# Two linear-attention heads at a time, then an MLP and a mixture of experts: weight halves and first rows made by VectorE, zero rows spread over pairs, 16-bit rank marks

## What is computed

```python
# attention: 4 x 8 heads, 576 positions, head size 64, 128 features
phi(x) = concat(exp(p), exp(-p)),  p = x @ w_phi - max|x @ w_phi|
kv = phi(k)^T v;  z = sum over positions of phi(k)
x  = (phi(q) kv) / (phi(q) z + 1e-6)              # 2304 tokens x 512
# MLP: 512 -> 2048 -> 512
h = x @ w_in;  y = (h * clip(h + 3, 0, 6) / 6) @ w_out
# mixture: 8 experts 512 -> 1024 -> 512, each token to its best expert
e = argmax(y @ w_gate); out = softmax(...)[e] * sigmoid(y @ w_output_gate)[e] * relu(y @ w1[e]) @ w2[e]
```

## Time and profile before

| | |
|---|---|
| median of three runs | 861.08 us |
| the profiled execution, its own time | 853.36 us |
| its span, first to last instruction | 851.8 us |
| TensorE matmul busy | 812.8 us, 95% |
| VectorE busy | 566.5 us, 67% |
| ScalarE busy | 388.9 us, 46% |
| GpSimd busy | 204.0 us, 24% |
| mean granted TensorE clock | 0.99 |

### The profile page before, as it was taken

One profiled execution on the slowest core, in us unless ns is written; L12 is line 12 of the kernel. 1 busy time (PEld: TensorE's weight loads), 2 busy tenths in 40 slices (PEclk: granted clock), 3 DMA queues, 4 the chain that ended last, 5 costly groups with the idle time before them and its releaser, 6 DMA issues.

```text
span 851.8 us, 19379 instructions
## 1 busy us (share of the span) xinstructions
PE 812.8 (95%) x7122; PEld 511.2 (60%) x7123; DVE 566.5 (67%) x1142; ACT 388.9 (46%) x843; POOL 204.0 (24%) x217
## 2 busy tenths in 40 slices
PE   6999989997899999999999999999998999999995
PEld 5666656664455455455455455456677777777773
DVE  5777878885887988998898898854732453222221
ACT  5877678883556546555555555533211121111110
POOL 4446579991000001001001001010121222111100
PEclk9999999999899999999999999999999999999998
DMA  7456866646263864955765855485263852565610
GB/s 230 148 195 195 250 198 205 196 139 213 89 233 133 262 213 173 260 223 174 246 222 197 234 222 210 136 343 178 100 220 105 321 208 79 227 223 221 223 65 13
DMA packets 67453, 164.41 MB, mean 193 GB/s; under 512 B 28614, under 2 KB 32966, under 8 KB 60736
## 3 DMA queue, kind: packets, MB, share of 16 engines
q1 hardware_dynamic: 61472, 146.74, 50.9%
q0 software_dynamic: 5760, 16.80, 5.6%
q10 hardware_dynamic: 160, 0.07, 0.0%
HBM read 114.16 MB, written 47.55 MB: 190 GB/s over the span
## 4 chain that ended last, share of the span: by engine, by line
PE 63%; DVE 18%; issue 7%; DMA 6%; ACT 2%; SPq 2%; POOL 1%; DVEq 0%; ACTq 0%; POOLq 0%
PE ps L900 14%; PE ps L995 13%; PE ps L983 13%; PE ps L889 12%; DVE arena L1556 3%; PE ps L749 3%; DVE u_mx L1529 3%; DMA recs<-rec 2%; PE ps L805 2%; PE ps L777 2%; DVE arena L1299 2%; DVE relu L1612 2%; DMA arena<-split 1%; PE ps L973 1%; DVE y_words L1521 1%
## 5 line engine op out<-in xcount | busy, mean ns | idle before, releaser
L889 PE MATMUL ps<-arena,w_in_sb 128*128 128x384 f16 x1152 | 201.8, 327 | 1.9 <-issue 1.9
L900 PE MATMUL ps<-w_out_sb,arena 128*128 128x512 f16 x576 | 172.7, 382 | 10.6 <-DVE stage L1617 10.6
L889 PEld LDWEIGHTS ps<-arena,w_in_sb 128*128 128x128 f16 x1152 | 112.5, 98 | 84.1 <-issue 3.6
L983 PE MATMUL ps<-x_t,arena 128*128 128x128 f16 x2112 | 121.5, 219 | 2.7 <-issue 2.7
L1276 ACT ACTIVATE x_t<-ps 128x512 f16<-128x512 f32 x54 | 31.6, 596 | 201.1 <-PE ps L983 175.8
L983 PEld LDWEIGHTS ps<-x_t,arena 128*128 128x128 f16 x2112 | 119.3, 98 | 6.6 <-issue 3.3
L995 PE MATMUL ps<-arena,x_t 128*128 128x512 f16 x528 | 117.9, 379 | 0.0
L900 PE MATMUL ps<-w_out_sb,stage 128*128 128x512 f16 x288 | 110.0, 382 | 0.0
L1248 ACT ACTIVATE arena<-relu 128x384 f16<-128x384 f32 x96 | 50.0, 520 | 116.3 <-DVE relu L1612 115.1
L900 PEld LDWEIGHTS ps<-w_out_sb,arena 128*128 128x128 f16 x576 | 55.8, 98 | 72.0 <-issue 15.0
L1099 ACT ACTIVATE arena<-ps,arena 128x128 f32<-128x128 f32 x288 | 79.8, 396 | 34.0 <-DVE arena L1301 24.1
(11 more groups left out here) (209 smaller groups left out, 949.7 us busy)
## 6 DMA issues: line engine op xcount, KB each, us to landing
arena<-split SPq DMA_DIRECT2D x36, 1024.0 KB, 5.8
arena<-in_moe_w SPq DMA_DIRECT2D x16, 2048.0 KB, 13.2
split<-arena SPq DMA_DIRECT2D x16, 2048.0 KB, 7.4
arena<-in_qkt SPq DMA_DIRECT2D x15, 576.0 KB, 6.6
stage<-in_moe_w_in SPq DMA_DIRECT2D x16, 512.0 KB, 5.4
stage<-in_moe_w_out SPq DMA_DIRECT2D x16, 512.0 KB, 6.4
x_t<-rows POOLq DMA_DIRECT2D x27, 257.0 KB, 3.0
y_words<-recs SPq DMA_DIRECT2D x32, 144.0 KB, 3.0
```

The source lines that it names most:

```text
L889: last = nc.tensor.matmul(ps[:, HB[f % GB], 0:BN], w_in_sb[:, lw, c, f * P:(f + 1) * P], xt[:, a, lx, c, :], start=c == 0 and lw + lx == 0 ...
L900: last = nc.tensor.matmul(ps[:, YB + r, :], g_sb[lg_][:, f % GB, r * P:(r + 1) * P], w_out_sb[:, lw, f, :], start=f == 0 and lg_ + lw == 0 ...
L983: last = nc.tensor.matmul(ps[:, bank, f % 4 * P:(f % 4 + 1) * P], w1_sb[b][:, lw, c, f * P:(f + 1) * P], xgt[:, a, lx, c, :], start=c == 0 ...
```

## The change

1. The high half of `w_in` is made by VectorE right before the low half (`piece_lo_of`, w = 0), no longer by GpSimd. In pair 14 this pair of operations moves from behind the scales to behind group 1 of the differences.
2. The first rows' high half is made by VectorE in one operation (`first_x`), no longer by ScalarE in two; the low half is one operation too. The last piece of `w_out` comes behind them.
3. `copy_low(u)` waits for the denominators of pair u-2 instead of u-1 (one semaphore for each buffer). VectorE takes the reciprocals of pair u-2 ahead of `copy_high(u)`, not behind it. ScalarE's loop starts two pairs later, the pairs before it are written out.
4. The zero rows go out one DMA in each pair from 8 to 15.
5. At the transition SyncE loads the second expert unit behind `rec_out(13)`, `rec_in(13)` and `den_over(15)`, not ahead of them.
6. GpSimd normalises up to pair 11 (before: 10). VectorE takes the reciprocals of pair 14 in chunk 1 of block 0 and those of pair 15 in chunk 4, with normalisations 12 and 13; 14 and 15 are in chunk 14.
7. The rank matmuls take a triangle, a square of ones and `onehot` in 16 bits.

```diff
-                if u == PAIRS // 2 - 1:
+                e = u - (PAIRS - E)
+                if e == 0:
                     sp.wait_ge(consts_made, 2)
-                    for e in range(E):
-                        sp.dma_start(rows[e * REGION:e * REGION + P, :], zrow).then_inc(pads_stored, 16)
+                if e >= 0:
+                    sp.dma_start(rows[e * REGION:e * REGION + P, :], zrow).then_inc(pads_stored, 16)
...
-            for m in range(2):
-                load_unit(0, m, m)
+            load_unit(0, 0, 0)
             rec_out(PAIRS - 3)
             rec_in(PAIRS - 3)
             den_over(PAIRS - 1)
+            load_unit(0, 1, 1)
...
             def last_pair():
                 sums_second(PAIRS - 1)
-                piece_hi_of(PAIRS - 1, 1)
-                normalise(PAIRS - 1 - BEHIND, 0)
+                for u in range(PAIRS - 1 - BEHIND, PAIRS - LAST):
+                    normalise(u, u % 2)
...
-                nc.tensor.matmul(ps[:, LB, 128:128 + BT * E], tri[:], rhs, start=True, stop=True)
-                nc.tensor.matmul(ps[:, LB, 192:192 + BT * E], ones[:], rhs, start=True, stop=True).then_inc(ranks_done, 1)
+                nc.tensor.matmul(ps[:, LB, 128:128 + BT * E], tri16[:], rhs, start=True, stop=True)
+                nc.tensor.matmul(ps[:, LB, 192:192 + BT * E], ones16[:], rhs, start=True, stop=True).then_inc(ranks_done, 1)
...
-                if not isinstance(u, int) or u > 0:
-                    act.wait_ge(den_moved, u * 16)
+                if not isinstance(u, int) or u > 1:
+                    act.wait_ge(den_moved[a], (u - a) * 8)
...
             def pair_out(u, a):
-                copy_high(u, a)
                 if not isinstance(u, int) or u > 1:
                     reciprocals(u - 2, a)
+                copy_high(u, a)
...
+                dst, cols = (w_in_flat, w_out_flat)[w], bass.ds((u - PAIRS // 2) * Q, Q)
+                if w == 0:
+                    dve.wait_ge(stage_loaded[a], (u - a) * 16 + 32)
+                    nc.vector.tensor_scalar(dst[:, 0, cols], stage[:, a, 0, :], s_up[:, 0:1], None, ALU.mult).then_inc(piece_hi, 1)
...
                 differences(u + 1, 1 - a, 1)
+                piece_lo_of(u, a, 0)
                 max_over_rows(1, 1)
                 differences(u + 1, 1 - a, 2)
                 max_of(1, slice(3, 4))
                 pair_out(u, a)
                 x_scales()
-                for w in range(2):
-                    piece_lo_of(u, a, w)
-                first_x_lo()
+                first_x()
+                piece_lo_of(u, a, 1)
...
+            def first_x():
+                dve.wait_ge(x_ready, DC)
+                nc.vector.tensor_scalar(xt[:, 0, 0], x_t[:, :, 0:BN], s_up[:, 3:4], None, ALU.mult).then_inc(xs_hi, 1)
+                x_lo(0, 0)
...
                     if f == 1 and not post:
-                        normalise(PAIRS - 5, 1)
-                        normalise(PAIRS - 4, 0)
+                        reciprocals(PAIRS - 2, 0)
+                    if f == 4 and not post:
+                        reciprocals(PAIRS - 1, 1)
+                        for u in range(PAIRS - LAST, PAIRS - 2):
+                            normalise(u, u % 2)
+                    if f == 14 and not post:
                         for u in range(PAIRS - 2, PAIRS):
-                            reciprocals(u, u % 2)
-                    if f == 4 and not post:
-                        normalise(PAIRS - 3, 1)
-                        normalise(PAIRS - 2, 0)
-                    if f == 14 and not post:
-                        normalise(PAIRS - 1, 1)
+                            normalise(u, u % 2)
```

More of the change, by code:

```diff
@@ L39 @@
 QUARTER = S // 4
-REP, WIDE, BEHIND = 32, 4, 5
+REP, WIDE, BEHIND, LAST = 32, 4, 5, 4
 GROUPS = [(8, 1), (0, 4), (4, 4)]
@@ L97, in moe_program @@
         ones = sb("ones", [P, P])
-        tri = sb("tri", [P, P])
+        ones16 = sb("ones16", [P, P], F16)
+        tri16 = sb("tri16", [P, P], F16)
         x_t = sb("x_t", [P, DC, N])
@@ L199, in moe_program @@
         r_b = sb("r_b", [P, BT, E])
-        onehot = sb("onehot", [P, BT, E])
+        onehot = sb("onehot", [P, BT, E], F16)
         r_s = sb("r_s", [P, 4, BT])
@@ L251, in moe_program @@
         high_copied = sem("high_copied")
-        den_moved = sem("den_moved")
+        den_moved = [sem(f"den_moved{a}") for a in range(2)]
         rec_made = sem("rec_made")
@@ L357, in pair_loop @@
             first()
-            both(0, 0, 0)
-            both(1, 1, 0)
-            with eng.Fori(1, PAIRS // 4) as i:
+            for u in range(4):
+                both(u, u % 2, 0)
+            with eng.Fori(2, PAIRS // 4) as i:
                 both(i * 2, 0, 0)
@@ L578, in later_constants @@
                 step(nc.gpsimd.tensor_copy(ident16[:], ident[:]))
-                step(nc.gpsimd.affine_select(out=tri[:], in_=ones[:], compare_op=ALU.is_ge, fill=0.0, base=-1,
+                step(nc.gpsimd.tensor_copy(ones16[:], ones[:]))
+                step(nc.gpsimd.affine_select(out=tri16[:], in_=ones16[:], compare_op=ALU.is_ge, fill=0.0, base=-1,
                                         pattern=[[1, P]], channel_multiplier=-1))
@@ L614, in normalise, with both @@
                 nc.gpsimd.tensor_tensor(x_of(u, 0, S), x_of(u, 0, S), rec_wide[:, bass.ds(u % WIDE * S, S)], ALU.mult).then_inc(x_ready, 1)
-            def both(u, a, phase):
+            def both(u, a):
                 sums_second(u)
-                if phase:
-                    piece_hi_of(u, a)
                 if u >= BEHIND:
@@ L633, in _ @@
             sums_first(1)
-            for u in range(1, PAIRS // 2):
-                both(u, u % 2, 0)
-            for u in range(PAIRS // 2, PAIRS - 1):
-                both(u, u % 2, 1)
+            for u in range(1, PAIRS - 1):
+                both(u, u % 2)
             last_pair()
@@ L1130, in x_hi @@
             def x_hi(n, b):
-                if isinstance(n, int) and n == 0:
-                    act.wait_ge(scale_step, X_UP)
-                    act.wait_ge(projected, PAIRS * 6)
-                    act.wait_ge(x_ready, DC)
-                else:
-                    first = isinstance(n, int) and n == 1
-                    act.wait_ge(x_ready, 2 * DC if first else PAIRS - BEHIND)
-                    if not first:
-                        act.wait_ge(x_last, BEHIND)
-                if isinstance(n, int) and n == 0:
-                    nc.scalar.activation(xt[:, b, 0, 0:2], x_t[:, 0:2, 0:BN], ACT.Copy, scale=s_up[:, 3:4]).then_inc(xs_half, 1)
-                    nc.scalar.activation(xt[:, b, 0, 2:DC], x_t[:, 2:DC, 0:BN], ACT.Copy, scale=s_up[:, 3:4]).then_inc(xs_hi, 1)
-                else:
-                    nc.scalar.activation(xt[:, b, 0], x_t[:, :, bass.ds(n * BN, BN)], ACT.Copy, scale=s_up[:, 3:4]).then_inc(xs_hi, 1)
+                first = isinstance(n, int) and n == 1
+                act.wait_ge(x_ready, 2 * DC if first else PAIRS - LAST)
+                if not first:
+                    act.wait_ge(x_last, LAST)
+                nc.scalar.activation(xt[:, b, 0], x_t[:, :, bass.ds(n * BN, BN)], ACT.Copy, scale=s_up[:, 3:4]).then_inc(xs_hi, 1)
             def parts(b):
@@ L1453, in x_scales @@
                 nc.vector.tensor_scalar(s_y[:], s_y[:], 1.0 / CG, None, ALU.mult).then_inc(x_scale, 1)
-            def first_x_lo():
-                for k, hi in ((0, xs_half), (2, xs_hi)):
-                    dve.wait_ge(hi, 1)
-                    last = nc.vector.scalar_tensor_tensor(out=xt[:, 0, 1, k:k + 2], in0=x_t[:, k:k + 2, 0:BN], scalar=s_up[:, 3:4],
-                                                          in1=xt[:, 0, 0, k:k + 2], op0=ALU.mult, op1=ALU.subtract)
-                last.then_inc(xs_lo, 1)
+            def first_x():
+                dve.wait_ge(x_ready, DC)
+                nc.vector.tensor_scalar(xt[:, 0, 0], x_t[:, :, 0:BN], s_up[:, 3:4], None, ALU.mult).then_inc(xs_hi, 1)
+                x_lo(0, 0)
             def x_lo(n, b):
```

16 lines of the change are left out of this document (3 added, 13 removed).

## The result

The changed kernel takes 852.27 us (median of 8 runs, 848.0 to 855.06) and the kernel before, run beside it, 859.88 us (8 runs, 857.72 to 862.28): a ratio of 0.9909, with an interval of 0.9884 to 0.9933, or some 7.6 us gained. The forecast was 846.8 us with 840 to 854. Direction and range hold, but of the 14.3 us forecast only about half came.

The account below looks back on a forecast made before the run. TensorE, busy 95% of the span, was taken as the bound, so its waits, slow running and cheaper matmuls set the end. 3.6 + 1.2 + 0 + 8.0 + 1.5 = 14.3 us off 861.1 gave 846.8 us, range 840 to 854.

Parts of the forecast that it names:

- The high half of `w_in`: Second-phase pairs: VectorE's high half 0.7 us, low half 2.26 to 1.28, pair 11.57 to about 11.25; 1.2 us gained.
- A: Rival: VectorE's high half costs 1.22 us, not 0.7; pairs take 11.8 us, total 851 us; chance 0.17.
- C: Rival: GpSimd keeps VectorE out between groups 1 and 2, pairs 8 to 14; high half 2.84 us, total 867; chance 0.05.
- The two pairs become ordinary: Two pairs from 106.62 to 132.71: ScalarE's 2.52 us wait and its slow matmuls go; 26.09 - 2 x 11.25 = 3.6 us gained.
- The zero rows and the looser wait: Pairs 8 to 15: spread zero-row DMAs and `copy_low`'s wait for an older move, both costed at nothing.
- The transition: Pair 14 to block 0's start: VectorE's and GpSimd's work changes but comes out even, 1 us better to 2 worse.
- 0.4 us sticking out: Pair 14: both `w_in` halves, about 2.0 us, fill VectorE's wait for turned maxima; some 0.4 us exceed it, delaying group 2.
- Block 0: First expert block: 5.64 us wait goes, with 2.8 us of slow clock, less 0.4 for VectorE in chunks 1 to 5; 8.0 gained.
- Rival B: Block 0's stall only moves: late `rec_out(13)` or VectorE behind in chunks 1 to 5; 851 to 854 us; chance 0.10.
- The step on `rec_out(13)`: Before block 0: store behind one 2 MB load lands after about half of 11.80 us, near 202; denominators there near 206.
- Ranks: Rank matmuls in six blocks: 0.37 us falls to 0.12 each, 1.5 us gained (0 to 2.2).
- worst case without a new mechanism: Whole kernel: all terms at their unfavourable bounds, 14.3 - 3.3 - 2 - 1.6 - 1.5 = 5.9 us gained.

Follow-up runs that it names:

- old kind: Four traces of the kernel before: first, unaltered rerun (858.48 us), longer ScalarE list (858.75 us), and only SyncE's order at the transition changed (855.45 us).
- changed kind: The ten other traces: the changed kernel twice (852.27, 853.87 us) and its variants with parts undone or GpSimd waits added (847.30 to 853.07 us).
- the gate in pair 8: Changed kernel plus one wait: in pair 8 GpSimd waits for the weights' scales before it normalises; 850.47 us, ratio 0.9913.
- The gate: Changed kernel plus one wait: after the last pair's sums GpSimd waits for VectorE's first rows and last low half before normalising; 851.55 us, ratio 0.9939.
- before run again: The kernel before, unaltered, run for a second trace; 858.48 us, ratio 0.9991.
- both gates: Changed kernel plus both GpSimd waits, for the weights' scales in pair 8 and for VectorE's last operations before block 0; 847.30 us, ratio 0.9889.
- the second measurement: The changed kernel, unaltered, timed again and traced a second time; 853.87 us, ratio 0.9952, 4.2 us gained.

## Why the prediction was right, and where its sum was not

**The high half of `w_in`: right.** 0.74 us against 0.7, the low half 1.28 against 1.28, the pair 11.35 against 11.25. Rivals A (1.22) and C (2.84) did not occur in the ordinary pairs. Undoing it alone gave 11.59 us and 2.27. Four pairs gave 46.16 - (11.36 + 3 x 11.35) = 0.75 us, where I had 1.2: the term was 0.1 us a pair too large. Against the other three traces of the old kind (46.3 us) it is 0.9.

**"The two pairs become ordinary": the step that failed.** The old wait for ScalarE went, as said. I forecast 3.6 us from it. The stretch from group 1 of pair 7 to that of pair 10 was 13.79 + 11.07 + 15.02 = 39.9 us in before's first trace and 14.98 + 14.20 + 11.33 = 40.5 in the changed kernel's: nothing gained. Over all traces without a gate it is 40.5 us on the mean of the four of the old kind and 39.1 of the six of the changed kind, so 1.4 us gained. The three with the gate in pair 8 have 36.0: with it the step would have gained 4.5, of which the part that is the clock's varies from one execution to the next. I had asked what the removed high half frees on GpSimd, and answered it for ordinary pairs only (the normalisation comes earlier, ahead of VectorE). In pair 8 the high half also carried a wait for the scales, and that wait held the normalisation off VectorE just while it made them. Take the instruction out and its wait goes with it. This is rival C's mechanism, at a place where I had not looked: not the high half but an operation of three elements was kept out, for 1.32 us instead of 0.17.

The Trainium skill's page "SBUF — State Buffer" (section "SBUF: two separate sides") says that a VectorE operation in a two-port mode, or one with two inputs in SBUF, and one of GpSimd exclude each other for a whole instruction; the one that starts first has the ports. The ends in the first trace agree with it (106.24 behind 106.21, 107.60 behind 107.57). I had weighed that rule for the long instructions alone.

**The zero rows and the looser wait: right at nothing.** Neither the spread DMAs nor the older move is seen anywhere, and each alone is enough.

**The transition: forecast even, within -1 and +2; it lost 1.0 us.** 197.54 - 179.50 = 18.04 us, where before had 17.04. The microsecond was lost ahead of the first rows: VectorE came to them 190.30 - 179.50 = 10.80 us into the stretch, where before was at the same point after 188.62 - 178.87 = 9.75. I had 0.4 us sticking out. The term left out what the new place does to the copy L1345, 1.13 us instead of 0.22 because it now starts behind a sum of GpSimd. The sign of it stood in the earlier trace rows, where the same line took 1.16 us in pair 7; I had read it for the high halves only. In all ten traces of the changed kind it takes 1.09 to 1.13 us and TensorE waits some 0.8 us for ScalarE in the last pair (here at 189.66); in the four of the old kind it takes 0.21 or 0.22 and that wait is absent. Neither gate covers this place, and no run took it out. From there to the last operation VectorE took 7.1 us, before 7.2, so that part was even, but by luck: I had the three operations at 1.0 + 1.9 + 1.28 = 4.2 us, and they took 1.86 + 2.85 + 2.43. I had GpSimd's two normalisations in the sum (2.8 us) but not what they do to VectorE beside them: they took 5.01 themselves. The gate shows it, with 4.96 us on VectorE and no wait ahead of block 0.

**Block 0: right in place, and near in size.** The wait of 5.64 us, the slow clock behind it and the two long operations are gone, in all traces of the changed kind (S to T is 393.3 to 393.8 us in every one). Rival B did not occur. S to T fell by 402.1 - 393.4 = 8.7 us against the first trace, and by 7.0 against before run again; five blocks' ranks are in it (1.5), so block 0 gave 5.5 to 7.2 us. I forecast 8.0, from the one trace I had. The step on `rec_out(13)` held roughly: store issued at 197.55, what waits for it at 204.34. Either edit alone removes the wait.

**Ranks: right.** 0.37 - 0.06 = 0.31 us, in six blocks 1.9, where I had 0.25 and 1.5.

**The stage of the experts: not in my sum at all, and mis-seen.** I took the profiled execution of before as typical and laid 7.7 us on top of it for the median. Some 4 us of that are one stop of ScalarE which that trace lacked and the others have (T to end 253.8 against 257.7 to 259.8 in the other three traces of the old kind). On top of it the six traces of the changed kind with the wait of 2.0 us in pair 8 take 258.7 to 263.2 us there, 260.5 on the mean, 1.8 us more than those three. TensorE, in the changed kernel's first trace, and then one row of its second:

```profile
609.09 2.75 PE L984 MATMUL ps<-arena,x_t 128*128 128x512 f16 x12 [2.46 <-DVE x_t L1702]
...
637.77 5.53 PE L972 MATMUL ps<-x_t,arena 128*128 128x128 f16 x96 [3.52 <-issue]
650.77 5.53 PE L972 MATMUL ps<-x_t,arena 128*128 128x128 f16 x96 [1.84 <-issue]
```

```profile
636.23 7.15 PE L972 MATMUL ps<-x_t,arena 128*128 128x128 f16 x96 [3.52 <-issue]
```

The waits ahead of L972 are where an expert's weights are first used. Two things differ between the kinds. One is the clock: 96 such matmuls take 5.53 us at 2.4 GHz, and behind the first of these waits they took 7.0 to 7.2 in nine of the ten traces of the changed kind and in one of the four of the old. The changed kernel's first trace is the exception, its second lost 1.6 us here and 1.7 at the slots before; by this lower clock the six lose 1.6 us on the mean and the three of the old kind 0.5. The other is the second wait, 1.7 to 2.2 us in eight of the ten and at most 0.5 in the old kind. An earlier arrival at a stream of weights that is no faster would lengthen it, but the marks don't bear that out: with the lower clock's part taken off, the second wait ends 58.9 to 60.2 us behind T in all eight, though T lies anywhere from 583.1 to 591.0. The kernel with both gates reaches that stage 7.8 us ahead of the changed kernel's first trace and ends 4.9 ahead, but 3.2 us of its stage are the lower clock; against the second trace it is 4.6 us ahead at the start and 5.3 at the end. No run varied the stream, and what makes the second wait longer and the lower clock more frequent stays open.

**The account,** by means over the six traces of the changed kind with the wait of 2.0 us in pair 8 and the four of the old kind, without before's first trace where it differs. Gained: pairs 7 to 10 1.4 us, ordinary pairs 0.9, S to T (block 0 and ranks) 400.65 - 393.6 = 7.1. Lost: transition 1.0, experts 1.8 (258.7 to 260.5, the last block's ranks in it), and 1.0 up to pair 7 (92.9 to 93.9 us), which I can't put down to the change: in part it is twelve matmuls near 11 us, which took 2.4 to 2.8 us instead of 1.5 in all six, but also in before again. That is 5.6 us, between the two timed gains of 7.6 and 4.2. Against the sum of 14.3: 2.2 us are missing at pair 8, 1.0 at the transition, 0.3 in the ordinary pairs, some 2.1 in blocks and ranks (7.1 for 9.25 with five blocks' ranks), 2.1 in the experts' stage and 1.0 ahead of pair 7. The prediction's worst case without a new mechanism was 5.9 us; the second measurement's 4.2 is below it. So the range held with luck: the ordinary pairs, the waits that went and the ranks were foreseen, but more than half of the missing time comes of GpSimd beside VectorE, of the lower clock and of a stage that the sum left out.

The steps that were wrong are thus two of the same kind, the removed wait in pair 8 and the small copy in pair 14, and one of method, the single trace.

## What to carry to other kernels

When an instruction moves from one engine to another, list the waits that it carried: whatever was queued behind it was held by them too, and may have been held off something that matters. Costs of GpSimd against VectorE are read by whether two instructions overlap, and the smallest operations of a chain that others wait for suffer most, so hold the GpSimd work that nobody needs yet behind that chain. Here two waits of one line each brought the kernel from 853.9 to 847.3 us in one group, the best version here. And a single trace of before is no base for a stage's length: compare a stage's marks over two or more executions before a sum is made on them, and look at the granted clock before a longer stage is put down to anything else.

## What the runs showed of the hardware that I had not expected

- An operation of VectorE on 128x3 elements, 0.17 us alone, took 1.32 us when it started 0.11 us behind the start of a GpSimd tensor_tensor of 1.40 us, and ended 0.03 us behind it. A copy of 128 elements on one partition, 0.22 us, took 1.13 when it started 0.23 us behind one of 1.28 us.
- Two long operations beside each other pay on both sides: GpSimd's two normalisations took 5.01 us instead of 2.77 and VectorE's two low halves 5.28 instead of 3.10.
- After an idle time of 2.0 us TensorE's granted clock was 0.51 (1.2 GHz) for 7 us in one execution and 1.00 (2.4 GHz) in another of the same kernel. At the same place it fell in five of six traces behind 2.0 us and in three of eight behind 0.87 us; ahead of block 0, behind 1.9 us, in one of eleven.
- A pair of rank matmuls of 24 columns in 16 bits costs the stream 0.06 us, where the 32-bit pair cost 0.37.
- ScalarE stopped for 5.1 to 5.6 us in the experts' stage at one and the same operation in all traces but one, whatever the kernel, with no releaser in the trace.
